# Powers and mask behind the first chunk's loads only, query decays spread by TensorE, and one index load two steps sooner

## What is computed

```python
# 1 linear attention with a decay per head; B=2, H=8, S=768, D=64, lam between 0.97 and 0.99
intra = (q_b @ k_b^T) * lam**(i-j) for i>=j          # "decay mask"
inter = (q_b * lam**(i+1)) @ kv_state                # "query decay"
out_b = intra @ v_b + inter
kv_state = lam**block * kv_state + (k_b * lam**(block-1-j))^T @ v_b
# 2 dense MLP on the 1536 tokens of 512 columns, hidden 2048
h = x @ w_in;  y = max(0.01*h, h) @ w_out
# 3 mixture of experts, 8 experts, hidden 1024, one expert for each token
e = argmax(y @ w_gate + bias[modality]);  out = gate * (relu(y @ w1[e]) @ w2[e])
```

## Time and profile before

| | |
|---|---|
| median of three executions | 498.42 us (497.13 to 500.88) |
| the profiled execution | 500.88 us |
| its span, first to last instruction | 499.2 us |
| TensorE busy | 482.1 us, 97% |
| GpSimd, VectorE, ScalarE busy | 207.2 us, 194.1 us, 180.9 us |
| mean DMA rate | 107 GB/s |

### The profile page before, as it was taken

One profiled execution on the slowest core, in us unless ns is written; L12 is line 12 of the kernel. 1 busy time (PEld: TensorE's weight loads), 2 busy tenths in 40 slices (PEclk: granted clock), 3 DMA queues, 4 the chain that ended last, 5 costly groups with the idle time before them and its releaser, 6 DMA issues.

```text
span 499.2 us, 8755 instructions
## 1 busy us (share of the span) xinstructions
PE 482.1 (97%) x2878; PEld 387.1 (78%) x2879; DVE 194.1 (39%) x416; ACT 180.9 (36%) x309; POOL 207.2 (42%) x222
## 2 busy tenths in 40 slices
PE   7799999999999999999999999999998999999993
PEld 7678788787878888887788888878886887888850
DVE  3543333333355522223462356747321392222210
ACT  0242343334253443444534565622222372222210
POOL 3775655544435448443544765322212171211000
PEclk9999999999999999999999999999999999999998
DMA  5995444332011350000930000140478648111100
GB/s 191 366 307 173 139 138 148 126 127 53 1 43 43 117 221 0 0 0 0 291 132 0 2 0 0 42 107 23 146 250 255 209 149 265 48 42 42 42 1 22
DMA packets 32763, 53.17 MB, mean 107 GB/s; under 512 B 8935, under 2 KB 20847, under 8 KB 32736
## 3 DMA queue, kind: packets, MB, share of 16 engines
q1 hardware_dynamic: 27312, 46.03, 29.0%
q0 software_dynamic: 2544, 6.77, 4.1%
q10 hardware_dynamic: 2880, 0.02, 0.3%
HBM read 46.40 MB, written 6.61 MB: 106 GB/s over the span
## 4 chain that ended last, share of the span: by engine, by line
PE 89%; DMA 5%; issue 2%; DVE 1%; ACT 1%; ACTq 0%; POOL 0%; SPq 0%; POOLq 0%; DVEq 0%
PE psum L1406 9%; PE psum L1414 9%; PE psum L1408 9%; PE psum L1416 9%; PE psum L1407 9%; PE psum L1415 9%; PE psum L1497 4%; PE psum L1499 4%; PE psum L1498 4%; PE psum L1477 4%; PE psum L1479 4%; PE psum L1478 3%; PE psum L1346 3%; PE psum L1369 2%; PE psum L1487 2%
## 5 line engine op out<-in xcount | busy, mean ns | idle before, releaser
L610 POOL TENSOR_TENSOR wi_lo<-wd_raw,wi_hi 128x512 fp32r<-128x512 f32 x48 | 62.1, 1295 | 132.7 <-ACT wi_hi L768 132.7
L1406 PE MATMUL psum<-xT,wi_lo 128*128 128x512 f32 x192 | 76.7, 399 | 0.0
L1414 PE MATMUL psum<-act_lo,wo_hi 128*128 128x512 f32 x192 | 75.6, 394 | 0.4 <-DVE act_lo L1023 0.4
L1408 PE MATMUL psum<-xT,wi_hi 128*128 128x512 f32 x192 | 74.9, 390 | 0.0
L1416 PE MATMUL psum<-act_hi,wo_hi 128*128 128x512 f32 x192 | 74.8, 390 | 0.0
L1407 PE MATMUL psum<-xT,wi_hi 128*128 128x512 f32 x192 | 74.8, 389 | 0.0
L1415 PE MATMUL psum<-act_hi,wo_lo 128*128 128x512 f32 x192 | 74.7, 389 | 0.0
L1020 DVE SCALAR_TENSOR_TENSOR act_f<-psum,act_f 128x512 f32<-128x512 f32 x48 | 33.1, 689 | 91.1 <-ACT act_f L786 90.7
L615 POOL TENSOR_TENSOR wo_lo<-wd_raw,wo_hi 128x512 fp32r<-128x512 f32 x48 | 62.9, 1310 | 2.2 <-ACT wo_hi L773 2.2
L786 ACT ACTIVATE act_f<-psum 128x512 f32<-128x512 f32 x48 | 28.6, 597 | 92.6 <-PE psum L1408 92.6
L1023 DVE TENSOR_TENSOR act_lo<-act_f,act_hi 128x512 fp32r<-128x512 f32 x48 | 33.9, 706 | 33.5 <-ACT act_hi L788 33.5
(11 more groups left out here) (207 smaller groups left out, 726.9 us busy)
## 6 DMA issues: line engine op xcount, KB each, us to landing
we_raw<-w_exp SPq DMA_DIRECT2D x40, 512.0 KB, 5.4
qk_in<-attn_qk SPq DMA_DIRECT2D x10, 512.0 KB, 4.0
kv_in<-attn_kv SPq DMA_DIRECT2D x10, 512.0 KB, 3.5
wd_raw<-w_dense SPq DMA_DIRECT2D x16, 256.0 KB, 3.1
x_d<-x_r SPq DMA_DIRECT2D x12, 256.0 KB, 4.0
wd_raw<-w_dense SPq DMA_DIRECT2D x16, 128.0 KB, 2.9
wd_raw<-w_dense SPq DMA_DIRECT2D x32, 64.0 KB, 2.8
qk_more<-attn_qk SPq DMA_DIRECT2D x2, 512.0 KB, 7.1
```

The costliest lines, as they stand in the source:

```text
L610: nc.gpsimd.tensor_tensor(wi_lo[:, r, :], dense_raw(f, 0), wi_hi[:, r, :].bitcast(F32), ALU.subtract).then_inc(s_wil, 1)
L1406: nc.tensor.matmul(h, w_lo, hi, start=(c == 0), stop=False)
L1408: mm = nc.tensor.matmul(h, w_hi, hi, start=False, stop=(c == DC - 1))
L1414: nc.tensor.matmul(bank(ACC + c), hi, act_lo[:, r, :], start=first, stop=False)
```

## The change

There are five edits.

1. On SP, `load_qk(1, 1)` moves from before the powers to behind the mask, and the two `q_decay` loads are gone.
2. `q_decay` is now made on the chip: POOL clears `of_head` (8 x 512) and sets it to ones where a row's head is that of the column (two `affine_select`), four TensorE multiplications spread the powers over the partitions into bank 7, and ScalarE copies them to `q_decay`.
3. On TensorE the order becomes `scores(0)`, the four multiplications, a wait for ScalarE's copy (bank 7 is used again), `warm(18)`, and only then `scores(1)`. `WARM` is (6, 18).
4. POOL waits for the copy (`s_tables` of 1) instead of the two loads.
5. On ScalarE the request for the numbers of tile 5 moves from behind `relu(3, 1)` to behind `rows(3)`.

```diff
@@ -30,7 +30,7 @@
 WSEM = 4
 WLOAD = 64
 ORDER = (0, 1, 4, 5, 2, 3, 6, 7)
-WARM = (6, 13)
+WARM = (6, 18)
 E = 8
 FE = 1024
 FC2 = FE // P
@@ -115,6 +115,7 @@
         state = place("state", [P, PAIRS, D], F32)
         state_dec = place("state_dec", [P, PAIRS, D], F32)
         pw = place("pw", [H, PWW], F32)
+        of_head = place("of_head", [H, PAIRS, P], F32)
         fill = place("fill", [P, (SLOTS + PAD) // P, 2], I32)
         zrow = place("zrow", [1, DM], F32)
         place = Placer(share_off, share_off + SHARE)
@@ -303,7 +304,9 @@
         s_pow = sem("powers_made")
         s_pow_d = sem("powers_in_dram")
         s_mask = [sem(f"decay_mask_loaded{i}") for i in range(2)]
-        s_tables = sem("query_decay_loaded")
+        s_qp = sem("query_decay_spread")
+        s_tables = sem("query_decay_ready")
+        s_head = sem("head_select_made")
         s_fill = sem("scratch_filled")
         s_qk = [sem(f"qk_loaded{u}") for u in range(LEAD)]
         s_kv = [sem(f"kv_loaded{u}") for u in range(LEAD)]
@@ -422,7 +425,6 @@
             sp.dma_start(pw[:, P + 1:P + 2], lam.rearrange("(h a) -> h a", a=1)).then_inc(s_in, 16)
             load_qk(0, 0)
             load_kv(0, 0)
-            load_qk(1, 1)
 
             sp.wait_ge(s_pow, 1)
             sp.dma_start(pow_d, pw[:]).then_inc(s_pow_d, 16)
@@ -430,10 +432,7 @@
             for half in range(2):
                 sp.dma_start(decay_mask[:, half::2, :], bass.AP(tensor=pow_d.tensor, offset=half * PWW + 1,
                                                                 ap=[[1, P], [2 * PWW, PAIRS], [1, P]])).then_inc(s_mask[half], 16)
-            for hp in range(2):
-                sp.dma_start(q_decay[hp * D:(hp + 1) * D],
-                             bass.AP(tensor=pow_d.tensor, offset=hp * PWW + P + 1,
-                                     ap=[[0, D], [2 * PWW, PAIRS], [1, P]])).then_inc(s_tables, 16)
+            load_qk(1, 1)
             load_kv(1, 1)
             for n in range(2, LEAD):
                 load_qk(n, n)
@@ -556,11 +555,17 @@
         @block.gpsimd
         def _(pool):
             nc.gpsimd.memset(ident[:], 0.0).then_inc(s_chain, 1)
+            nc.gpsimd.memset(of_head[:], 0.0).then_inc(s_head, 1)
             nc.gpsimd.memset(before[:], 1.0).then_inc(s_chain, 1)
             nc.gpsimd.memset(ones[:], 1.0).then_inc(s_chain, 1)
             pool.wait_ge(s_chain, 3)
             nc.gpsimd.affine_select(out=ident[:], in_=ident[:], compare_op=ALU.not_equal, fill=1.0, base=0,
                                     pattern=[[-1, P]], channel_multiplier=1).then_inc(s_chain, 1)
+            pool.wait_ge(s_head, 1)
+            for hp in range(2):
+                nc.gpsimd.affine_select(out=of_head[:, :, hp * D:(hp + 1) * D], in_=of_head[:, :, hp * D:(hp + 1) * D],
+                                        compare_op=ALU.not_equal, fill=1.0, base=-hp,
+                                        pattern=[[-2, PAIRS], [0, D]], channel_multiplier=1).then_inc(s_head, 1)
             nc.gpsimd.affine_select(out=before[:], in_=before[:], compare_op=ALU.is_gt, fill=0.0, base=0,
                                     pattern=[[1, P]], channel_multiplier=-1).then_inc(s_chain, 1)
             pool.wait_ge(s_chain, 5)
@@ -599,7 +604,7 @@
             pool.sem_inc(s_qd, 1)
             pool.sem_inc(s_sd, 1)
             decay_k(0, 0, 0, 16)
-            pool.wait_ge(s_tables, 32)
+            pool.wait_ge(s_tables, 1)
             for n in range(1, LEAD):
                 decay_q(n, n % 2, n, 16)
                 decay_k(n, n % 2, n, 16)
@@ -752,6 +757,8 @@
 
         @block.scalar
         def _(act):
+            act.wait_ge(s_qp, 1)
+            nc.scalar.activation(q_decay[:].rearrange("p a n -> p (a n)"), bank(7), ACT.Copy).then_inc(s_tables, 1)
             act.sem_inc(s_eh, 4 * FC2)
             act.sem_inc(s_ids, 16 * (PRE - 1))
             act.sem_inc(s_ids2, 16 * (PRE - 1))
@@ -899,12 +906,12 @@
             hid(2, 0)
             relu(2, 1)
             rows(3)
+            act.wait_ge(s_idc, PRE + 2)
+            load_ids(ids_n, PRE + 2, s_ids)
             hid(2, 1)
             relu(3, 0)
             hid(3, 0)
             relu(3, 1)
-            act.wait_ge(s_idc, PRE + 2)
-            load_ids(ids_n, PRE + 2, s_ids)
             with act.Fori(PRE, last) as t:
                 rows(t + 1)
                 k1 = act.value_load(tab[0:1, bass.ds(FI_ + 1 + t, 1)], min_val=0, max_val=E)
@@ -1386,13 +1393,18 @@
             pe.wait_ge(s_chain, 4)
             warm(WARM[0])
             scores(0, 0, 16, score_bank(0))
+            pe.wait_ge(s_head, 3)
+            pe.wait_ge(s_pow, 1)
+            for hp in range(PAIRS):
+                mm = nc.tensor.matmul(bank(7)[:, hp * P:(hp + 1) * P], of_head[:, hp, :], pw[:, P + 1:2 * P + 1], start=True, stop=True)
+            mm.then_inc(s_qp, 1)
+            pe.wait_ge(s_tables, 1)
+            warm(WARM[1])
             for n in range(LEAD):
                 if n + 1 < LEAD:
                     if n > 0:
                         pe.wait_ge(s_pr, 2 * n)
                     scores(n + 1, n + 1, 16, score_bank(n + 1))
-                if n == 0:
-                    warm(WARM[1])
                 attend(n, n % 2, n, 16, out_bank(n), first=(n == 0), shared=False)
             pe.wait_ge(s_chain, 5)
```

## The result

The changed kernel takes 497.0 us in the median of 20 executions (495.4 to 501.5). The kernel before, run beside it on the same chip, takes 499.7 us in the median of 20 (497.1 to 503.7). The ratio is 0.9939, with a 95% interval of 0.9914 to 0.9963: a gain of 3.0 us, between 1.8 and 4.3 (the two medians differ by 2.7 us). That is within 1%, as forecast, and inside the range. The forecast of 496.2 us started from 498.4 us, the median of three executions; with 20 the starting point is 1.3 us higher and the gain 0.8 us larger than the forecast's 2.2 us.

The account below looks back on a forecast made before the run. Transfers were taken to set the pace up to 20 us, and TensorE after that. The late -1.8 us and the front -0.4 us sum to -2.2 us, from the 498.4 us median to 496.2 us; range 494.4 to 499.3 us.

Parts of the forecast that it names:

- The late term: Late tiles: moving tile 5's request removes TensorE's wait for gathered rows, -1.8 us, bounds 0 and -2.
- The front term: Front: `scores(3)` starts at 19.6 or 20.1 instead of 20.09; -0.4 us, bounds -0.9 and +0.8.
- 1.6 us for 512 KB: SP's queue: price of a 512 KB transfer, from 256 KB of query decays and two 512 KB transfers in 4.0 us.
- The 3.7 us taken over for the last two loads: SP's queue: chunk 3's `qk` again lands 3.7 us after chunk 2's.
- the load at 19.6: Front: chunk 3's `qk` lands at 19.6 and lets `scores(3)` start then.
- the forecast's lower bound: Front: -0.9 us, if a 512 KB transfer takes less than 1.6 us.
- the fast case: Front: the four multiplications run at the fast clock level, 1.1 us and not 2.0; `scores(3)` could start at 19.2.
- Warm multiplications at the lower clock: Rival, front: the 36 warm instructions take 7.9 us, 3.8 us more; +2.1 us in all, 500.5 us; chance 10%.
- The late wait stays or moves: Rival, late tiles: tile 5's gather takes over 10.2 us or a later wait grows; 498.0 us; chance 12%.
- The table load comes between: Rival, front: ScalarE's 1.28 us table load delays its copy and `scores(1)`; 497.5 us; chance 8%.
- the argument with the single wait: ScalarE, front: the copy has one wait where the old first activation had two, so the table load can run in the idle start.

Follow-up runs that it names:

- the late edit alone: The kernel before with only the request for tile 5's numbers moved behind `rows(3)`; 497.93 us, ratio 0.9946.
- the front alone: The changed kernel with the request for tile 5's numbers put back behind `relu(3, 1)`; 498.08 us, ratio 0.9972.
- decays from memory: The changed kernel with `q_decay` loaded from DRAM again, behind the mask, without `of_head`, its multiplications and the copy; 498.85 us, ratio 0.9956.
- the repetition: The changed kernel once more, without an edit; 496.20 us, ratio 0.9935 against the kernel before.
- the queue's order undone: The changed kernel with `load_qk(1, 1)` ahead of the powers again; 497.45 us, ratio 0.9954.
- the scatter's: The changed kernel with POOL's scatter put ahead of the last piece of its split of an expert's weights; 496.88 us, ratio 0.9959.
- the free warm ones: The changed kernel with the 18 warm multiplications ahead of the wait for ScalarE's copy, into PSUM bank 2; 496.14 us, ratio 0.9929.

## Why the prediction was right

**The late term held.** Forecast -1.8 us, measured 14.27 - 12.34 = 1.93 us at its place and 2.0 over the late stretch; the late edit alone removes the wait and the front alone brings it back. The steps: the request was put at 358.0 and left at 356.24, the gather at 370.6 and left at 369.24. About 1.1 us of each difference is the front's gain, which moves all later work. POOL does issue it right behind the `xg_m` gather (367.17), as the step said.

**The front term had the right sign and was too small.** Forecast -0.4 us, bounds -0.9 and +0.8; measured -1.2 at `scores(3)` and -1.1 at the mark, beyond the lower bound. The step that was mis-sized is "1.6 us for 512 KB". By it `qk 1`, `qk 2` and the load of chunk 3 land at 12.6, 15.9 and 19.6 (its own sum gives 15.8 for the second); they landed at 12.1, 14.6 and 17.2. The value came from a stretch that holds the query decays too, and charged all of it by the byte. The landings one by one, issue plus time to landing from the lists of transfers, in us:

| | before | changed | decays from memory |
| --- | --- | --- | --- |
| second half of the mask (by DVE's use of it) | 12.3 | 10.9 | 11.0 |
| first load of 512 KB behind it | 15.1 | 12.1 | 13.7 |
| second | 16.3 | 13.4 | 15.1 |
| third | 17.6 | 14.6 | 16.3 |
| fourth | 20.0 | 15.9 | 17.5 |
| fifth | 21.6 | 17.2 | 18.8 |

Ordinary loads of 512 KB land 1.2 to 1.3 us apart, up to the third in the kernel before as well. The 256 KB of decays put 2.8 us and not 1.2 between the mask and the first load, so they cost about 1.6 us, twice what the price by the byte gave them, in both kernels that load them. Whether that time goes into the transfer of their short pieces or into issuing them (1.36 us on SP) is not separated. The 3.7 us taken over for the last two loads is no fixed price: such a gap, 3.6 to 3.9 us, stands in five of the 14 traces, three of them with the new front, and in the others it is 2.5 to 2.9 us. With either, the changed kernel's load would land before the 18.90 at which TensorE came to `scores(3)`. So TensorE's row and not the load at 19.6 set `scores(3)`, which is the case of the forecast's lower bound, and that row was worked out well: 19.2 for the fast case, 18.90 measured.

**TensorE's row, step by step.** Start 2.4 (2.38), though `of_head` is cleared behind `ident` and not ahead of it; what it delays is the step that makes `ident` from it. `scores(0)` at 5.4 (5.24). The four multiplications 1.1 us in the fast case (1.15), end 8.5 (8.24). The copy with its hand-over 0.7 us (0.69). Warm 4.1 us (4.29). `scores(1)` at 13.3 (13.14). `scores(2)` at 16.0 (15.72). The powers confirmed at 6.2 (mask issued at 6.03). No idle time before `scores(2)` and `scores(3)`, as forecast.

**Warm multiplications at the lower clock (10%).** Not in the traces: the 36 took 4.29 us, 0.119 us each, and `scores(1)` started far ahead of 16.0. The lower level itself is real in this front: it came after 2.04 and 2.31 us of idle time in the late-only kernel, after 2.31 us in the one with decays from memory, and after 4.07 us without warm ones. The copy's 0.69 us stayed well short of that. The rival may still describe some executions: 5 of 20 of the changed kernel took 500.0 to 501.5 us, against 495.4 to 497.8 for the others, and 2 of 12 in the repetition took 500.0. So did 3 of 12 in each of two further kernels with 18 warm ones behind the copy (the queue's order undone, 499.9 to 501.9, and the scatter's, 500.0 to 501.6). This is about the rival's 3.8 us, and none of the 31 executions with 13 warm ones, or with the 18 beside the copy, was above 498.6. Against it stands the granted clock of whole executions: of the five, two have 0.997 and none is under 0.994, while the faster ones have 0.991 to 0.997. That is weak evidence, since the granted clock stood at full in the kernel before, too, while the first nine instructions of its warm stretch took 0.22 us each. No profile fell on such an execution, so what makes them slow stays open.

**The late wait stays or moves (12%).** It did not stay: the gather leaves 10.3 us before the rows are needed at 379.6. Nor did the next one take its place: the request of tile 6 leaves at 377.91, its gather at 381.84, and the next distance is 12.3 us.

**The table load comes between (8%).** It did not: it ran at 0.85, in ScalarE's idle start, as the argument with the single wait had it, and the copy follows TensorE's last multiplication at once. It took 1.28 us both times. The Trainium skill ("ScalarE: Activation LUTs", What ACT_TABLE_LOAD costs) gives that figure too. The further 1380 ns that it names for a drain do not show: before, the activation followed 1.30 us after the load's start, and in the changed kernel nothing waited for the load, so that trace could not show them.

**What the forecast could not see.** It rested on one execution of the kernel before. Three traces of the old front have the mark at 27.9, 29.1 and 30.6; seven of the new kind of front (the changed kernel twice, the front alone, 13 warm ones twice, the free warm ones, the scatter's) have it at 26.1 to 27.0. The old late wait was 1.6, 1.8 and 4.1 us; with the request sooner it is nought in all eleven traces that have it. The change takes two places out of the reach of slow transfers. This is not what made the forecast too small: between the first two profiles, one of them the forecast's own, the gain is 3.1 us already (1.1 and 2.0), and its excess over 2.2 us is the 0.7 us of the front and the 0.1 to 0.2 us of the late term. How much the slow executions of the old kernel add to the median is not shown; the two further traces of its front are of the slowest executions beside them, and between the worse of these, span 502.4, and the changed kernel it is 6.4 us. The page "TensorE: Matmul & The Clock Gate" (Part 1) of the Trainium skill says that runs of one kernel differ in how many matmuls run slow at the start. The traces agree: with the same instructions ahead of it, `scores(0)` took 2.08 us in both traces of the kernel before and 1.16 in the late-only one, and 1.39 to 2.08 us in the ten with the new front.

## What to carry to other kernels

When a request stands just before its use, its wait in one profile is a sample (1.6, 1.8 and 4.1 us here); a change that gives it several microseconds of margin takes away the mean over executions, so look at two or three profiles before pricing it. A price for transfers is read from the landings of equal transfers one by one, not from a stretch that mixes several kinds. Work taken off a transfer queue and put on TensorE pays as long as TensorE's row ends behind the loads that now land sooner; compare the two, load by load. Filler multiplications are there to bridge the wait for the first load: leaving them out cost 1.4 us here in the traces by the lower clock (0.8 us by the medians), twice as many cost 3.7 us in the trace, and between 13 and 18 nothing could be measured in the medians.

## What the hardware showed that was not expected

- The write of the powers, 8 KB, which SP must see confirmed, took 1.3 to 1.6 us in the ten traces with one chunk's loads ahead of it (4.56 to 6.03 in the changed kernel), and 3.0, 3.2, 4.3 and 4.4 us in the four with one load of 512 KB more ahead.
- TensorE kept the full clock over idle stretches of 0.69, 1.38, 1.50 and 1.94 us at the front and 1.8 us in the late tiles, and came to the lower level after 2.04, 2.31 (in two kernels), 4.07 and 4.1 us. After 2.31 us in the kernel with decays from memory, the next `scores` still ran mostly at the full level and the fall came behind it. In the late-only kernel the full level was back about four microseconds after work began again.
- A request of 1 KB of row numbers took 5.57 us in one execution and 7.07 us in another, beside the loads of weights.
